# One attention and two expert layers on one core: the first pass of the last layer fed by masked combine weights, ahead of the sorting

## The reference

```python
x = local_attention(q, k, v, mem_k, mem_v)       # 4 batches x 8 heads x 768 rows, chunks of 32
# soft mixture, 4 slots for each of 8 experts: 32 slots
logits = x @ phi
d = softmax(logits, axis=0); slot_in = d.T @ x    # (32, 512)
slot_out[e] = relu(slot_in[e] @ w1m[e]) @ w2m[e]
c = softmax(logits, axis=1); x = c @ slot_out     # c: the "combine" weights, (3072, 32)
# top-1 layer
logits = x @ w_gate; e_idx = argmax(logits, axis=1)
gate_w = softmax(logits)[e_idx]; eom = sigmoid(x @ w_output_gate)
out[mask_e] = gate_w * eom[:, e] * (relu(x[mask_e] @ w1[e]) @ w2[e])
```

## Time and profile before

| | |
|---|---|
| median of 3 runs | 503.69 us |
| lowest, highest | 502.85, 507.48 us |
| the profiled execution | 510.57 us |
| its span, first to last instruction | 508.7 us |
| mean granted TensorE clock | 0.982 |
| TensorE busy | 460.1 us, 90% of the span |
| DVE, ACT, POOL busy | 214.3, 273.5, 185.0 us |
| HBM read, written | 88.51 MB, 7.73 MB |

### The profile page before, as it was taken

How to read it: one execution, slowest core, us unless ns; L and a number is a source line. 1 busy time by engine, 2 the same in 40 slices (tenths; PEclk the granted TensorE clock), 3 DMA queues, 4 the chain that set the end, 5 groups by cost and what they waited for, 6 DMA issues and landing times.

```text
span 508.7 us, 12976 instructions
## 1 busy us (share of the span) xinstructions
PE 460.1 (90%) x4601; PEld 252.1 (50%) x4602; DVE 214.3 (42%) x890; ACT 273.5 (54%) x464; POOL 185.0 (36%) x147
## 2 busy tenths in 40 slices
PE   2798999999998799896799999999999999999992
PEld 2687777777776543363543434343434343434330
DVE  1678988988988461038421212121212121212110
ACT  1466876776775410103225666565656565666540
POOL 2568877877877210002301222222222222222110
PEclk9999999999999999998969999999999999999998
DMA  9879999999999987999999775101010101010000
GB/s 149 152 238 194 254 276 183 275 272 172 273 278 229 381 263 268 422 428 429 406 383 403 295 289 188 45 22 44 23 44 22 44 22 44 23 44 22 22 2 0
DMA packets 98651, 95.66 MB, mean 188 GB/s; under 512 B 86680, under 2 KB 87128, under 8 KB 95928
## 3 DMA queue, kind: packets, MB, share of 16 engines
q1 hardware_dynamic: 94328, 73.38, 51.9%
q10 hardware_dynamic: 1008, 14.68, 7.4%
q0 software_dynamic: 3280, 7.15, 4.0%
HBM read 88.51 MB, written 7.73 MB: 189 GB/s over the span
## 4 chain that ended last, share of the span: by engine, by line
PE 60%; DMA 14%; SPq 11%; POOL 6%; issue 5%; ACT 2%; DVE 1%; POOLq 0%; ACTq 0%; DVEq 0%
PE bank L897 39%; DMA arena<-in_moe_w_dram 11%; PE bank L874 6%; POOL arena L541 3%; POOL arena L536 3%; SPq L406 3%; PE bank L675 2%; SPq L396 2%; DMA arena<-in_mem_v_dram 2%; PE bank L607 2%; SPq L408 2%; SPq L399 2%; PE bank L819 1%; PE bank L863 1%; PE bank L622 1%
## 5 line engine op out<-in xcount | busy, mean ns | idle before, releaser
L897 PE MATMUL bank<-arena 128*64 (+1 forms) x448 | 205.8, 604 | 0.0
L907 PE MATMUL bank<-arena 128*64 128x512 f32 x448 | 205.8, 604 | 0.0
L897 PEld LDWEIGHTS bank<-arena 128*64 128x64 f32 x448 | 57.5, 138 | 104.3 <-issue 99.3
L575 POOL DMA_INDIRECT out_dram<-arena,tok_sorted x28 | 28.4, 1013 | 194.4 <-ACT arena L1307 194.4
L1152 DVE TENSOR_SCALAR arena<-bank 128x256 f32<-128x256 f32 x112 | 39.7, 418 | 104.5 <-PE bank L874 104.5
L536 POOL TENSOR_TENSOR arena<-arena,row_inv 96x1024 f32<-96x1024 f32 x32 | 60.6, 1893 | 32.3 <-DVE row_inv L974 32.3
L541 POOL TENSOR_TENSOR arena<-arena,row_max 96x1024 f32<-96x1024 f32 x32 | 60.6, 1893 | 12.7 <-DVE row_max L981 12.7
L981 DVE CUSTOM_DVE_ANT_0 arena<-bank,masks 96x128 f32<-96x128 f32 x256 | 55.0, 277 | 9.7 <-PE bank L607 9.7
L907 PEld LDWEIGHTS bank<-arena 128*64 128x64 f32 x448 | 57.5, 138 | 0.0
L1332 ACT COPY arena<-arena 128x2048 f32 x27 | 51.2, 1898 | 9.3 <-issue 9.3
L1327 ACT COPY arena<-arena 128x2048 f32 x27 | 51.3, 1900 | 1.6 <-issue 1.3
(11 more groups left out here) (180 smaller groups left out, 577.0 us busy)
## 6 DMA issues: line engine op xcount, KB each, us to landing
arena<-in_moe_w_dram SPq DMA_DIRECT2D x18, 2048.0 KB, 10.2
arena<-in_moe_w_dram ACTq DMA_DIRECT2D x7, 2048.0 KB, 9.5
arena<-in_moe_w_dram SPq DMA_DIRECT2D x24, 512.0 KB, 8.3
arena<-in_v_dram SPq DMA_DIRECT2D x32, 240.0 KB
arena<-in_q_dram SPq DMA_DIRECT2D x32, 192.0 KB, 4.6
arena<-in_k_dram SPq DMA_DIRECT2D x20, 192.0 KB, 4.1
arena<-in_moe_w_dram SPq DMA_DIRECT2D x2, 1024.0 KB, 8.4
arena<-in_k_dram SPq DMA_DIRECT2D x4, 240.0 KB
```

The lines of the kernel that those rows point to most:

```text
L897: mm(bank[4 + par][0:HR, :], h_t[:, par, lo:lo + HR], w2_all[:, bass.ds(at_w2 * SEG + f * DM, DM)], start=(f == 0), stop=(f == KF - 1))
L907: ins = mm(bank[4 + par][HR:TR, :], h_t[:, par, lo + HR:lo + TR], w, start=(f == 0), stop=(f == KF - 1))
```

## The change

- **Pass 0.** Expert 0 has at least two halves, so pass 0 is always its first 128 tokens. DVE sets `combine` to zero outside tile 0, and the one-hot product of this with the lane tables (TensorE, into bank 0), one copy by ACT and four small products with `fold` give the turned rows of pass 0: no sorting, gather, spread or transpose. `layer1(0)` follows at once.
- **Sorting** of the rest: its one-hot product stands behind `layer1(0)`, its join inside the wide products of pass 0; the gates' product and join stand behind them. DVE makes both spot tables, POOL none.
- **Folds** 0 and 1 stand ahead, 2 to 5 between pass 0 and pass 1, 6 and 7 inside passes 1 and 2. Weights come in the order w1[0], w1[1], w2[0], w1[2] to w1[7], w2[1] to w2[7], in other segments. Three second-layer matrices wait until all before have landed before; now five do.
- **Rows in DRAM** are numbered p*32+t, so a partition writes one piece of 4 KB; `row_sorted` is for gathers, and DVE computes `tok_sorted` for scatters from it. Pass j uses gather slot (j - 1) % 4.
- **`step2`**: `layer1(j + 1)` now stands ahead of the load of `half_expert`, which is in `layer2(j)`. The hardware loop covers passes 4 to 25.

```diff
-        place[("hidden", e)] = (5, 6, 7, 8, 9)[e % 5]
+        place[("hidden", e)] = (5, 6, 7, 1, 2, 5, 6, 7)[e]
         place[("w2", e)] = e
-    units += [("hidden", e) for e in range(EARLY_G + 1)] + [("w2", 0)]
-    units += [("hidden", e) for e in range(EARLY_G + 1, E)] + [("w2", e) for e in range(1, E)]
+    units += [("hidden", 0), ("hidden", 1), ("w2", 0)]
+    units += [("hidden", e) for e in range(2, E)] + [("w2", e) for e in range(1, E)]
...
-            pool.dma_start(c_dram[0:N].rearrange("(t p) s -> p t s", p=TQ), combine).then_inc(c_out, 16)
-            pool.dma_start(c_dram[N:N + 1], blank[:]).then_inc(c_out, 16)
-
-
-            pool.wait_ge(tile_found, 1)
-            g.tensor_tensor(spots[:, :, 0, :], spots[:, :, 1, :],
-                            token_no[:].unsqueeze(2).to_broadcast([TQ, NT, SPAN]), ALU.mult).then_inc(spot_found, 1)
+            pool.dma_start(c_dram[0:N].rearrange("(p t) s -> p t s", p=TQ), combine).then_inc(c_out, 16)
+            pool.dma_start(c_dram[N:N + NT], blank[:]).then_inc(c_out, 16)
...
-            for e in range(1, BEFORE_HOT):
-                hidden(e)
-
-
-            chunks = (3, 0, 1, 2)
+            hidden(1)
+
+
+            chunks = (0, 1, 3, 2)
...
-            pe.wait_ge(spot_found, 1)
-            one_hot(0, bank[2]).then_inc(hot_used, 1)
-            pe.wait_ge(hot_summed, 1)
-            mm(bank[1][:, 0:SPAN], hot_sum[:, 0, :], fold[:, :], start=True, stop=True).then_inc(sorted_made, 1)
-            for e in range(BEFORE_HOT, EARLY_G + 1):
-                hidden(e)
-            pe.wait_ge(gate_spots, 1)
-            one_hot(1, bank[5]).then_inc(gate_hot_used, 1)
...
+            pe.wait_ge(first_masked, 1)
+            hot_products(bank[0], combine).then_inc(first_summed, 1)
+            spin(bank[2], 3)
+            pe.wait_ge(first_copied, 1)
+            for i in range(4):
+                ins = mm(bank[1][NS * i:NS * (i + 1), 0:TR], fold[:, :], first_sum, start=True, stop=True)
+            ins.then_inc(c_turned, 1)
+            spin(bank[2], 3)
...
-            def step2(j, par, more, do_l1, do_turn, inside=None, first=False):
+            def layer2(j, par, more, first=False, inside=lambda f: None):
 
                 if first:
                     at_w2 = 0
                 else:
                     at_w2 = pe.value_load(half_expert[0:1, bass.ds(2 * j, 1)], min_val=0, max_val=E - 1)
-                if do_l1:
-                    layer1(j + 1, 1 - par, True)
                 pe.wait_ge(relu2_made, j + 1)
...
-            pe.wait_ge(tiles_known, 1)
-            turn(0, 0, False)
+            def step2(j, par, fold_inside=None):
+
+                def inside(f):
+                    if f == KF // 2:
+                        if fold_inside is not None:
+                            hidden(fold_inside)
+                        turn(j + 2, par, True)
+
+                layer1(j + 1, 1 - par, True)
+                layer2(j, par, True, inside=inside)
...
             layer1(0, 0, False)
+            pe.wait_ge(spot_found, 1)
+            hot_products(bank[5], spots[:, :, 0, :]).then_inc(hot_used, 1)
+            pe.wait_ge(g_copied, 2)
+            layer2(0, 0, False, first=True, inside=inside_0)
+            hidden(2)
+            pe.wait_ge(gate_spots, 1)
+            hot_products(bank[5], spots[:, :, 1, :]).then_inc(gate_hot_used, 1)
             turn(1, 1, True)
-            pe.wait_ge(g_copied, EARLY_G + 1)
-            for j in range(ONE_BY_ONE):
-                step2(j, j % 2, j >= 2, True, True, EARLY_G + 1 + j if EARLY_G + 1 + j < E else None, first=(j == 0))
-            with pe.Fori(ONE_BY_ONE // 2, (NP - 2) // 2) as i:
+            hidden(3)
+            join(1)
+            hidden(4)
+            pe.wait_ge(g_copied, 5)
+            layer1(1, 1, True)
+            hidden(5)
+            pe.wait_ge(gate_ready, 1)
+            layer2(1, 1, False, inside=inside_1)
+            step2(2, 0, 7)
+            step2(3, 1)
+            with pe.Fori(2, (NP - 2) // 2) as i:
                 for par in range(2):
-                    step2(i * 2 + par, par, True, True, True)
-            for j in range(NP - 2, NP):
-                step2(j, j % 2, True, j + 1 < NP, False)
+                    step2(i * 2 + par, par)
+            layer1(NP - 1, 1, True)
+            layer2(NP - 2, 0, True)
+            layer2(NP - 1, 1, True)
...
+            dve.wait_ge(c_out, 32)
+            vec.scalar_tensor_tensor(out=combine, in0=r_one[:, 6, :].unsqueeze(2).to_broadcast([TQ, NT, NS]), scalar=0.0,
+                                     in1=combine, op0=ALU.is_equal, op1=ALU.mult).then_inc(first_masked, 1)
```

More of the change, by code:

```diff
@@ L344, in g_bank @@
         def g_bank(e):
[L346 removed]
+            return (3, 4, 7, 3, 0)[e] if e < 5 else 7
         def live(b, t):
@@ L876, in layer1, with join @@
                 ins.then_inc(l1_made, 1)
-            def step2(j, par, more, do_l1, do_turn, inside=None, first=False):
+            def join(k):
+                pe.wait_ge(hot_summed, k + 1)
+                mm(bank[5][:, TR + k * SPAN:TR + (k + 1) * SPAN], hot_sum[:, k, :], fold[:, :], start=True, stop=True).then_inc(sorted_made, 1)
+            def layer2(j, par, more, first=False, inside=lambda f: None):
                 if first:
@@ L890, in step2 @@
                 for f in range(KF):
-                    if f == KF // 2:
-                        if inside is not None:
-                            hidden(inside)
-                        if do_turn:
-                            turn(j + 2, par, True)
+                    inside(f)
                     lo = f * 128
@@ L1299, in ct_copy @@
                 act.wait_ge(c_turned, j + 1)
-                sc.copy(c_t[:], bank[6][:, 0:TR]).then_inc(ct_copied, 1)
+                sc.copy(c_t[:], bank[6 if j else 1][:, 0:TR]).then_inc(ct_copied, 1)
             def evacuate(j):
@@ L1332, in fill_high @@
                 sc.copy(w2_second[j % 2][:, SEG // 2:SEG], w2_all[:, bass.ds(e * SEG + SEG // 2, SEG // 2)]).then_inc(second_high, 1)
+            g_copy(0)
+            pick(0)
+            act.wait_ge(lanes_ready, 1)
+            for t in range(HOT):
+                n = 3 * HOT + t
+                ins = sc.activation(hot_tok(3)[:, t, :], lane_no[:], ACT.Abs, bias=r_one[:, 7, n:n + 1], scale=-1.0)
+            ins.then_inc(lane_gaps, 1)
+            act.wait_ge(lane_gaps, 1)
+            sc.activation(hot_tok(3), hot_tok(3), ACT.Relu, bias=ones[0:TQ, 0:1], scale=-1.0).then_inc(hot_made_act, 1)
+            g_copy(1)
+            act.wait_ge(first_summed, 1)
+            sc.copy(first_sum, bank[0][:, 0:TR]).then_inc(first_copied, 1)
+            ct_copy(0)
+            act.wait_ge(gate_shifted, 2)
+            sc.activation(r_one[:, 3, :], r_one[:, 2, :], ACT.Exp, scale=-1.0).then_inc(gate_exped, 1)
             act.wait_ge(tiles_known, 1)
-            pick(0)
+            fill_low(1)
+            fill_high(1)
+            g_copy(2)
             pick(1)
-            ct_copy(0)
             ct_copy(1)
+            g_copy(3)
+            g_copy(4)
             act.wait_ge(gate_ready, 1)
-            fill_low(1)
-            for j in range(NP):
-                if EARLY_G + 1 + j < E:
-                    g_copy(EARLY_G + 1 + j)
+            evacuate(0)
+            pick(2)
+            fill_low(2)
+            g_copy(5)
+            ct_copy(2)
+            fill_high(2)
+            ct_copy(3)
+            g_copy(6)
+            pick(3)
+            evacuate(1)
+            fill_low(3)
+            for j in range(2, NP):
+                if j == 2:
+                    g_copy(E - 1)
                 if j + 2 < NP:
```

161 lines of the change are left out of this document (83 added, 78 removed).

## The result

| | before | after |
|---|---|---|
| median (lowest to highest) of 17 runs each | 507.31 us (501.86 to 508.55) | 512.06 us (508.64 to 517.32) |
| ratio to before, 95% interval | | 1.0117 [1.009, 1.0144] |
| the profiled execution, its span | 510.57, 508.7 us | 514.76, 513.0 us |
| first layer of pass 4 starts | 289.78 us | 287.13 us |
| first layer of pass 27 starts | 484.76 us | 488.98 us |

On 507.31 us the ratio is +5.9 us, between 4.6 and 7.3. The last two rows of the table split it in the profiled executions: the front ends 2.65 us earlier, and the 23 passes from there cost 201.85 us in place of 194.98, 6.87 more. Behind the last first layer both need 24 us.

A forecast was written before the change was run, and what follows sets the result against it. It took weight transfers to bound the kernel up to 244.7 us and TensorE from there. Front -1.0 and register load +5.6 gave +4.6 us on the 503.69 us median: 508.3 us, range 501 to 514.

The forecast's parts named there:

- case A: Whole kernel: the forecast itself, 508.3 us, with a range of its own of 505.5 to 511 us; chance 0.42.
- the side to which I gave 0.44: Whole kernel: slower by over 1% (5.0 us), which is above 508.7 us; chance 0.44.
- The load: Steady passes: register load behind the first layer delays the wide weights, 0.25 us a loop pass, 0.15 elsewhere; +5.6 us.
- the discount for a weight load under the product ahead: Steady passes: a weight load of 0.13 us can lie partly under the product ahead, so 5.9 us became 5.6.
- The upper bound of 0.45 a pass: Steady passes: index 0.1, load 0.65 and 0.25, less 0.5 to spare; 11 us, 513.7 us in all; chance 0.10.
- rival B: Steady passes: TensorE's queue hides the load, so only -1.0 us is left and the time is 502.7 us; chance 0.19.
- The front: Fold 1 to pass 4's first layer: 1.5 us gained, 0.5 set against it; -1.0 us, bounds -4.7 and +4.
- The clock: Front, in the hole behind fold 1: TensorE at half clock from 234.8 to some 241.6 us.
- the 0.5 us set aside for products handed over late: Front: three one-hot products might stand still, as the gate product did for 0.33 us; 0.5 us against the gain.
- Rival C: Front, 236 to 255 us: the clock stays at 0.50 past 241.6, costing 5 us; time 513 us; chance 0.17.
- Rival D: Front wins its whole 4.7 us and the loop loses nothing: 499.0 us; chance 0.12.
- The price of 1.7 us: First pass: the table on DVE beside POOL's multiply took 2.93 us, the other two 1.21 and 1.22.

The follow-up runs named there:

- the load early: The changed kernel with the load of half_expert ahead of the first-layer products again in passes 2 to 26: 505.15 us, ratio 0.9985.
- the filled old order: The kernel before with 11 idle products in its 2.96 us wait after fold 1 and 4 in its 1.23 us wait: 508.54 us, ratio 1.0009.
- the one with 14 idle products: The changed kernel with the load early and 14 idle products in the 5 us hole behind fold 1: 505.02 us, ratio 0.9942.
- the hole filled and the load early: The changed kernel with the load early and 20 idle products behind fold 1: 502.64 us, ratio 0.9907; run again, 502.55 us, ratio 0.9889.

## Why the prediction was right, and where it was not

The prediction was 508.3 on a median of 503.69, a ratio of 1.0092. The measured ratio, 1.0117 [1.009, 1.0144], holds it at its edge; on that median it is 509.6 us, within the 505.5 to 511 of case A. It is slower by a little over 1%, the side to which I gave 0.44, and not within 1%, to which I gave 0.47.

- **The load.** Forecast +5.6 us, as 0.25 a pass in the loop and 0.15 elsewhere; measured 0.30 and 0.20, 22 x 0.30 + 3 x 0.20 = 7.2 us, and 6.9 between the medians with the load late and early. The step was right, its size 1.3 to 1.6 us low. Of that 0.3 was the discount for a weight load under the product ahead; no such overlap is seen, since the short products are through when the weights come. The other 0.05 a pass is in the commands: from index to weights they take 1.05 us, where I had 1.03, and they start 0.29 us behind the array's start and not 0.27. (The upper bound of 0.45 a pass was off too: its own terms give 0.5.)
- **The queue** (rival B). It fell. The 64 of the Trainium skill (Advanced Engine Details and Errata, Engine Queue Depths) would have all of the first layer queued before the load. The page adds "complicated with tiling", which the prediction left out, and the products of the first layer are small tiles (32*128 in the rows). Here the sequencer passed the middle of it 0.02 us after the array had begun it and the end 0.29 us after it had begun the layer, and a second load behind it cost 0.66 us. Which count the queue holds stays open: the second 16 pairs of weight load and product were handed over in 0.27 us, about twice as fast as the array takes them (1.05 for 32), so a fixed count of commands alone does not give both times.
- **The front.** Forecast -1.0; -0.8 [-2.1, +0.6] with the load early. In the profiled pair it is -1.42 from fold 1 on, with some 0.3 us of the late load in it. The other 1.2 of the 2.65 lie ahead of fold 1 and say nothing: fold 0 of the changed kernel began at 225.07 us in one profile and at 220.88 in the other. Step by step: mask at 234.4 (forecast 235.2), each table 1.2 us, wide products from 246.3 (247.3), gate product to 257.4 (259), pass 4 at 287.1 (288.8). Nearly all of them run 1 us early since fold 1 did. That the term came out so near is in part luck, as the next point shows.
- **The clock** was at 0.50 for 10.24 us and not 6.8, from 233.3 to 243.5. From the first product to the first layer it cost 1.1 us more than forecast (3.7 for 2.6 between the product's end and the first layer, in idle and small products); the second product gave 0.8 back (1.9 for 2.7), and the 0.5 us set aside for products handed over late were not needed. How long the stretch is, one trace does not tell: the same kernel in its second profile had 13.65 us at 0.50 and needed 62.16 us from fold 0 to pass 4 in place of 62.06. The prediction also misread the kernel before. It put both stretches behind the long waits, and the second began 3.8 us before the wait of 1.23 us ended, behind a row of small ones. And it counted the 3.52 us of fold 2 among what there was to win, which the filled old order shows to be covered.
- **Rival C** did not happen in the two profiles of the changed kernel, but did in the one with 14 idle products. Its price holds as far as it can be compared: 5 us, counted from a stretch of 6.8 us. There it was 7.0 more than with a stretch of 3.41 us, about 0.5 us for each further us at half clock, which makes 5.2 from 6.8.
- **Rival D** (-4.7 for the front at full clock) was nearly right for a kernel that I had not thought of: with the hole filled and the load early the two comparisons give 4.7 and 5.6 us under the kernel before, and the profile 59.03 us from fold 0 to pass 4 for 63.89.
- **POOL.** The price of 1.7 us for its multiply beside the tables is confirmed in one execution, at the second table.

**What to carry to other kernels.** Before you move a command that the sequencer itself must finish (a register load, an index), look at how long the work queued ahead of it lasts on the array: the cover is a matter of the pieces' duration. The same 0.65 us are free behind pieces of 0.43 us, even twice; behind pieces of 0.033 they cost 0.2 us, 0.3 with an index, and a second load is paid in full. A new order of work is one thing and its register loads another; here undoing one line's place turned 1.2% slower into no change. And before you fill a wait to keep the clock up, look in the trace where the stretch at 0.50 begins and whether a wait behind it covers it; here filling most of the hole left the clock low in four executions of twelve, filling all but 0.34 us in none of 14.

## What the runs showed of the hardware that I had not expected

- The stretch at 0.50 in the front varies from kernel to kernel and from execution to execution without a change of the order: 3.4 us in one execution with the load early, 10.24 and 13.65 in two of the changed kernel, 17.07 in the one with 14 idle products, none in two with 20. Its length does not tell its price: 3.41 us under fold 2 cost the old order nothing.
- Two late loads cost more than twice one: 0.30 and then 0.66 a pass. The first, 0.76 us with its index, hides 0.46 us behind the short products, the second nothing.
- A load in the middle of a run of short products costs as much as one at its end (8.81 us a pass against 8.78 in the loop).
- A POOL multiply that ended 1.75 us behind the end of DVE's first table held DVE's second, 1.2 us alone, back to 2.91 us.
